# An attention and two-FFN kernel: v transposed by VectorE in blocks of 32, four H banks, FFN2's weights in 16 pieces

## The reference

```python
def reference(q, k, v, tau, moe_w_in, moe_w_out, moe_a, moe_b, moe2_w_in, moe2_w_out):
    # q, k, v: [1, 6016, 256]; w_in: [256, 2048]; w_out: [2048, 256]; all float32
    qn = q / (norm(q, axis=1) + 1e-6); kn = k / (norm(k, axis=1) + 1e-6)
    s = kn.transpose(0, 2, 1) @ qn / tau              # 256 x 256, over the channels
    a = exp(s - s.max(-1)); a /= a.sum(-1) + 1e-9
    x = (v @ a).reshape(6016, 256)
    h = x @ moe_w_in                                  # first FFN (FFN1)
    P = a0 + a1*h + a2*h**2 + a3*h**3
    Q = 1.0 + abs(b0)*abs(h) + abs(b1)*h**2
    x = (P / (Q + 1e-6)) @ moe_w_out
    h = x @ moe2_w_in                                 # second FFN (FFN2)
    return (h * clip(h + 3, 0, 6) / 6) @ moe2_w_out
```

## Time and profile before

| what | value |
|---|---|
| median of three executions | 1181.27 us |
| profiled execution, its time | 1181.6 us |
| its span, first to last instruction | 1179.4 us |
| mean granted TensorE clock | 0.988 of full speed |
| busy share of the span | PE 97%, weight loads 83%, DVE 74%, ACT 75%, POOL 64% |
| chain that ended last | PE 92%, DVE 3%, ACT 2%, POOL 1%, issue 1% |
| start (q, k, softmax, first fold piece) | 0 to 64.9 us |
| step 0 (FFN1 of block 0 alone) | 64.9 to about 134 us |

### The profile page before, as it was taken

How to read it: one execution, slowest core, us unless ns; L and a number is a source line. 1 busy time by engine, 2 the same in 40 slices (tenths; PEclk the granted TensorE clock), 3 DMA queues, 4 the chain that set the end, 5 groups by cost and what they waited for, 6 DMA issues and landing times.

```text
span 1179.4 us, 17866 instructions
## 1 busy us (share of the span) xinstructions
PE 1140.6 (97%) x6058; PEld 975.1 (83%) x6058; DVE 877.7 (74%) x1258; ACT 880.1 (75%) x1463; POOL 749.6 (64%) x596
## 2 busy tenths in 40 slices
PE   7887799999999999999999999999999999999998
PEld 6765688888888888888888888888888888888887
DVE  6768888877877877777777777777787777777721
ACT  6577788877777777777777777777787787787743
POOL 2157567766666666666666666666666666666643
PEclk9889999999999999999999999999999999999999
DMA  9731000000000000000000000000000000000000
GB/s 320 277 123 34 1 1 19 15 1 19 1 19 19 1 19 19 2 19 19 1 18 19 2 19 18 1 18 19 1 19 18 1 19 1 1 19 1 1 18 18
DMA packets 15961, 34.19 MB, mean 29 GB/s; under 512 B 1792, under 2 KB 6144, under 8 KB 15616
## 3 DMA queue, kind: packets, MB, share of 16 engines
q1 hardware_dynamic: 15872, 33.04, 7.8%
HBM read 26.87 MB, written 6.16 MB: 28 GB/s over the span
## 4 chain that ended last, share of the span: by engine, by line
PE 92%; DVE 3%; ACT 2%; POOL 1%; issue 1%; DMA 0%; SPq 0%; POOLq 0%; DVEq 0%; ACTq 0%
PE H L367 15%; PE H L369 14%; PE H L368 14%; PE OP L491 7%; PE OP L493 7%; PE OP L495 7%; PE YP L367 7%; PE YP L368 7%; PE YP L369 7%; PE OP L376 4%; DVE SQ L783 1%; PE H L407 1%; POOL SQ L324 1%; PE OP L430 1%; DVE g_hi L776 1%
## 5 line engine op out<-in xcount | busy, mean ns | idle before, releaser
L324 POOL TENSOR_TENSOR SQ<-SQ,AB 128x512 f32<-128x512 f32 (+1 forms) x192 | 244.5, 1273 | 360.5 <-ACT SQ L586 320.3
L336 POOL TENSOR_TENSOR g_lo<-R,g_hi 128x512 fp32r<-128x512 f32 (+1 forms) x192 | 246.1, 1282 | 28.6 <-ACT g_hi L617 28.6
L584 ACT ACTIVATE AB<-H,absb 128x512 f32<-128x512 f32 (+1 forms) x192 | 130.3, 679 | 158.1 <-PE H L369 156.9
L330 POOL TENSOR_TENSOR g_lo<-SQ,Y 128x512 fp32r<-128x512 f32 (+1 forms) x192 | 245.1, 1277 | 1.7 <-DVE SQ L791 1.7
L491 PE MATMUL OP<-wd_hi,g_hi 128*128 128x256 f32 x752 | 211.9, 282 | 0.6 <-POOL g_lo L336 0.6
L493 PE MATMUL OP<-wd_lo,g_hi 128*128 128x256 f32 x752 | 211.8, 282 | 0.0
L761 DVE TENSOR_TENSOR T<-T,H 128x512 f32<-128x512 f32 (+1 forms) x192 | 129.5, 674 | 108.8 <-ACT T L592 108.8
L495 PE MATMUL OP<-wd_hi,g_lo 128*128 128x256 f32 x752 | 209.6, 279 | 0.0
L776 DVE SCALAR_TENSOR_TENSOR g_hi<-H,coef,Y 128x512 fp32r<-128x512 f32 (+1 forms) x192 | 141.9, 739 | 76.0 <-ACT Y L605 75.7
L367 PE MATMUL YP<-g_hi,wd_hi 128*128 128x512 f32 (+1 forms) x384 | 154.4, 402 | 14.0 <-POOL g_lo L330 12.1
L611 ACT ACTIVATE R<-H 128x512 f32<-128x512 f32 (+1 forms) x192 | 113.6, 591 | 69.8 <-PE H L369 68.6
(11 more groups left out here) (83 smaller groups left out, 2188.7 us busy)
## 6 DMA issues: line engine op xcount, KB each, us to landing
qk<-in_q SPq DMA_DIRECT2D x23, 256.0 KB, 7.1
qk<-in_k SPq DMA_DIRECT2D x23, 256.0 KB, 8.2
v_raw<-in_v SPq DMA_DIRECT2D x11, 512.0 KB, 3.5
out<-o_tok SPq DMA_DIRECT2D x11, 512.0 KB, 2.6
w_raw_b<-in_moe_w_out SPq DMA_DIRECT2D x8, 512.0 KB, 6.1
w_raw_a<-in_moe_w_in SPq DMA_DIRECT2D x1, 2048.0 KB, 13.0
w_raw_b<-in_moe_w_in SPq DMA_DIRECT2D x4, 512.0 KB, 6.9
v_raw<-in_v SPq DMA_DIRECT2D x1, 384.0 KB, 13.5
```

The source lines that it names most:

```text
L324: nc.gpsimd.tensor_tensor(SQ[:, j % 4, 0:w], SQ[:, j % 4, 0:w], AB[:, j % 2, 0:w], ALU.add)\
L330: nc.gpsimd.tensor_tensor(g1_lo[:, j % 4, 0:w], SQ[:, j % 4, 0:w], Y[:, j % 2, 0:w], ALU.mult)\
L336: nc.gpsimd.tensor_tensor(g2_lo[:, j % 4, 0:w], R[:, j % 4, 0:w], g2_hi[:, j % 4, 0:w].bitcast(fp32), ALU.subtract).then_inc(g2_lo_done, 1)
L584: nc.scalar.activation(AB[:, j % 2, 0:w], h, ACT.Abs, scale=absb[:, 0:1])
```

## The change

- **v.** `load_v` brings a block in eight transfers of 32 partitions, in runs of 32 floats (128 bytes), so that each 32x32 square lies where the square of the transposed block belongs. `v_transpose` then transposes inside the squares, one VectorE instruction for 128x512, SBUF to SBUF, in chunks 5 and 8 (`V_AT`). ACT makes `vT_hi`, POOL `vT_lo`. TensorE's `transpose_v`, the two places in the ring and DVE's `vT_split` go. Also for block 0: its transposes now come after the copy of probT on DVE.
- **Banks.** One tile `H` with four banks. FFN1 takes banks 0 and 1, FFN2 banks 2 and 3; in step 0 FFN1 has all four. `up1` of chunk j waits for `rest` of chunk j-2, `up2` for `gate2` of chunk j-2.
- **Lags.** `LAG_DOWN1` is 3 (was 2), so `SHIFT2` is 4 (was 3).
- **Weights.** FFN2's weights have their own buffers and are split in 16 pieces of 128x512, in slots of steps 0 and 1 (slot = 16 t + j). Their loads wait for no split, and stand behind block 1 of v in SP's queue. `PIECES` is eight folds of 256 columns (was 2 of 256 and 3 of 512).
- **GpSimd's order in a chunk.** `q_body(j)`, `g2_split`, `vT_split`, a piece of weights, `quotient_lo(j-1)`. The wait for `product` is gone. `R` has two buffers (was four).
- Tokens of a block are stored in rows of 128 tokens, not four neighbours to a partition.

```diff
-    LAG_DOWN1 = 2
+    LAG_DOWN1 = 3
-    V_BEHIND = 7, 10
-    W_SLOTS = 0, 6
-    RING = 3
+    V_AT = 5, 8
+    WU2_AT = 2, 6, 10, 11, 12, 13, 15, 23
+    WD2_AT = 14, 16, 17, 18, 19, 27, 29, 30
-    PIECES = [2, 2, 4, 4, 4]
+    PIECES = [2] * 8
-        R = sb("R", [P, 4, W], fp32)
+        R = sb("R", [P, 2, W], fp32)
-        H1, H2, YP, OP = ps("H1", RING), ps("H2", 1), ps("YP", 2), ps("OP", 2)
+        H, YP, OP = ps("H", 4), ps("YP", 2), ps("OP", 2)
...
+        def h1(t, j):
+            turn = 4 if isinstance(t, int) and t == 0 else 2
+            return H[:, j % turn, 0:width(t)]
+
+        def wait_h1(engine, t, j):
+            if isinstance(t, int) and t == 0:
+                if j >= 4:
+                    wait_chunk(engine, rest_done, (0, j - 4))
+            elif isinstance(t, int) and t == 1 and j < 2:
+                wait_chunk(engine, rest_done, (0, J - 4 + j))
+            else:
+                wait_chunk(engine, rest_done, back(t, j, 2))
...
             def load_v(blk):
                 m = width(blk) // P
-                sp.wait_ge(vT_psum, CT * blk)
-                sp.dma_start(v_raw[:, 0:m, :], tokens_of(v[0], blk, m)).then_inc(v_in, 16)
+                sp.wait_ge(vT_done, CT * blk)
+                rows = tokens_of(v[0], blk, m).rearrange("(a q) (h b r) -> h b q a r", q=32, h=CT, b=4)
+                to = v_blocks[:, :, 0:m * P].rearrange("p h (a r) -> p h a r", r=32)
+                for c in range(CT):
+                    for b in range(4):
+                        sp.dma_start(to[32 * b:32 * (b + 1), c], rows[c, b]).then_inc(v_in, 16)
...
             sp.dma_start(w_raw_a[:], w_up_h[0]).then_inc(w1_in, 16)
-            sp.dma_start(v_raw[:, 0:tiles_of[0], :], tokens_of(v[0], 0, tiles_of[0])).then_inc(v_in, 16)
+            load_v(0)
             load_v(1)
-            for k in (1, 2):
-                for part in range(4):
-                    load_weight(k, part)
+            for part in range(4):
+                load_wu2(part)
+            for part in range(4):
+                load_wd2(part)
...
+            def vT_split(blk, c, par):
+                w = width(blk)
+                pool.wait_ge(vT_hi_done, CT * blk + c + 1)
+                low_half(vT_lo[par][:, c, 0:w], vT_raw[par][:, c, 0:w], vT_hi[par][:, c, 0:w]).then_inc(vT_lo_done, 1)
...
             def step(t, par):
                 for j in range(J):
-                    y = stage(t, j - LAG_DIVIDE)
                     if exists(t):
-                        if y:
-                            wait_chunk(pool, product_done, y)
                         q_body(t, j)
-                    if y:
-                        quotient_lo(*y)
                     if x := stage(t - 1, j - SHIFT2):
                         g2_split(*x)
-                    if isinstance(t, int) and t == 0:
-                        for k in (1, 2):
-                            if W_SLOTS[k - 1] <= j < W_SLOTS[k - 1] + 4:
-                                weight_lo(k, j - W_SLOTS[k - 1])
+                    if j in V_AT and exists(t) and exists(t + 1):
+                        vT_split(t + 1, V_AT.index(j), 1 - par)
+                    if slot(t, j) in WU2_AT:
+                        wu2_split(WU2_AT.index(slot(t, j)))
+                    if slot(t, j) in WD2_AT:
+                        wd2_split(WD2_AT.index(slot(t, j)))
+                    if y := stage(t, j - LAG_DIVIDE):
+                        quotient_lo(*y)
...
-                for i in range(m):
-                    done = nc.tensor.transpose(H1[:, b, i * P:(i + 1) * P], v_raw[:, i, c * P:(c + 1) * P], ident[:])
-                done.then_inc(vT_psum, 1)
...
+            def v_transpose(blk, c, par):
+                w = width(blk)
+                if c == 0:
+                    dve.wait_ge(v_in, 128 * (blk + 1))
+                    if exists(blk - 2):
+                        wait_chunk(dve, u1_done, (blk - 2, J - 1))
+                nc.vector.transpose(vT_raw[par][:, c, 0:w], v_blocks[:, c, 0:w]).then_inc(vT_done, 1)
 
             dve.wait_ge(probT_psum, 1)
             nc.vector.tensor_copy(probT, YP[:, :, 0:C]).then_inc(probT_ready, 1)
             for c in range(CT):
-                vT_split(0, c, 0)
+                v_transpose(0, c, 0)
...
             def step(t, par):
                 for j in range(J):
+                    if j in V_AT and exists(t) and exists(t + 1):
+                        v_transpose(t + 1, V_AT.index(j), 1 - par)
                     if j == LAG_DOWN1 and exists(t - 1):
                         yT_split(t - 1)
```

More of the change, by code:

```diff
@@ L103, in attention_ffn_ffn @@
         small = sb("small", [P, 48], fp32)
[L104 to L106 removed]
+        v_blocks = sb("v_blocks", [P, CT, W], fp32)
         o_tok = sb("o_tok", [P, BT, C], fp32)
@@ L145, in attention_ffn_ffn @@
         w1_in, v_in = map(sem, ("w1_in", "v_in"))
-        wb_in = [sem(f"wb_in_{i}") for i in range(4)]
+        wd1_in, wu2_in, wd2_in = ([sem(f"{x}_in_{i}") for i in range(4)] for x in ("wd1", "wu2", "wd2"))
         ident_ready, ones_ready, absb_ready = map(sem, ("ident_ready", "ones_ready", "absb_ready"))
@@ L210, in every_step, with wait_h2, wu2_unit, wd2_unit @@
                 body(t, t % 2)
[L213 to L237, removed]
-        def h2(blk, j):
-            last = isinstance(blk, int) and blk == NB - 1
-            return (H1 if last and j % 2 else H2)[:, 0, 0:width(blk)]
+        def h1(t, j):
[9 more added lines that the diff above has]
+                wait_chunk(engine, rest_done, back(t, j, 2))
+        def h2(blk, j):
+            return H[:, 2 + j % 2, 0:width(blk)]
+        def wait_h2(engine, blk, j):
+            if isinstance(blk, int) and blk == 0 and j < 2:
+                wait_chunk(engine, rest_done, (0, J - 2 + j))
+            else:
+                wait_chunk(engine, g2_done, back(blk, j, 2))
+        def wu2_unit(u):
+            at = u // 2 % 2 * F + u // 4 * (F // 2) + u % 2 * UNIT
+            return slice(at, at + UNIT)
+        def wd2_unit(u):
+            return slice(u * UNIT, (u + 1) * UNIT)
+        def slot(t, j):
+            return t * J + j if isinstance(t, int) else None
         def stage(t, at):
@@ L436, in up1 @@
                 w = width(t)
-                wait_bank(pe, t, place(j))
+                wait_h1(pe, t, j)
                 if j == 0:
@@ L463, in up2 @@
                 w = width(blk)
-                if at := back(blk, j, 2 if isinstance(blk, int) and blk == NB - 1 and j else 1):
-                    wait_chunk(pe, g2_done, at)
-                if j == 0 and isinstance(blk, int) and blk == 0:
-                    pe.wait_ge(split_lo, 8)
+                wait_h2(pe, blk, j)
+                if isinstance(blk, int) and blk == 0 and j in (0, J // 2):
+                    pe.wait_ge(wu2_lo_done, 4 if j == 0 else 8)
                 cols = slice(j * P, (j + 1) * P)
@@ L591, in p_start @@
                 wait_chunk(act, t3_done, back(t, j, 2))
-                nc.scalar.activation(T[:, j % 2, 0:w], H1[:, bank(place(j)), 0:w], ACT.Identity, bias=A2, scale=A3)\
+                nc.scalar.activation(T[:, j % 2, 0:w], h1(t, j), ACT.Identity, bias=A2, scale=A3)\
                   .then_inc(t_done, 1)
@@ L818, in step @@
                         rest(*x)
-                    if j in V_BEHIND and exists(t) and exists(t + 1):
-                        vT_split(t + 1, V_BEHIND.index(j), 1 - par)
                     if exists(t):
```

166 lines of the change are left out of this document (81 added, 85 removed).

## The result

The changed kernel takes 1162.1 us (median of 4 runs, 1161.0 to 1164.5) against 1181.4 (1180.1 to 1181.5). The ratio is 0.984, 95% interval [0.9825, 0.9859]. The sign was right, the size was not.

What follows compares the result with a forecast made beforehand. PE was taken to bound seven eighths of the profile, step 0's latency chain an eighth. -8.6 - 0.6 - 3.2 + 2.6 = -9.8 took 1181.6 to 1171.8 us; forecast 1166 to 1177 (0.60), range 1163 to 1180.

Steps and rivals of the forecast that it cites:

- the sum for step 0: Step 0: 16 x 3.45 plus 0.8, pieces 8 x 0.45, folds 0.5 x 6, v 1.65; 64.4 us, 3.2 gained.
- The rival that I gave 0.13: Step 0's chain gets shorter if `product` and `q_body` don't exclude each other: step 60 us, time 1163 to 1167; chance 0.13.
- Transposes off PE: Steps 1 to 10: 20 groups of four transposes leave PE, 0.43 us each, 8.6 us gained.
- FFN2's bank: FFN2's two banks: `up2` no longer waits for the `gate2` right before; half of PE's 1.25 us wait, 0.6 us gained.
- Two banks cost nothing in the loop: FFN1 on two banks in the loop: 2.75 us of slack before `up1` takes up the delays of `rest`; cost 0.
- The lags: One more chunk passes before PE is full: cost 2.6 us, bounds 0 and 5.
- The start: Before the first `up1`: v's new path is done by 63 us and hidden by 1.9 us; no cost.
- The small packets: v's loads in packets of 128 bytes: 6 to 50 ns each, 25 taken, nothing lost.
- the rival of the late v: v's packets over 50 ns lengthen ACT's wait in chunk 2; from 93 ns on the kernel is slower; chance 0.05.
- `q_body` first makes it slower: Step 0 and ramp: a late DVE finds `q_body` running and loses 1.0 us, 4.0 a chunk; 1185.5 us; chance 0.10.
- The start didn't eat the gain: Rival: ACT's stall, the dear ramp and late v eat the gain; 1176 to 1180 us; chance 0.10.
- the mean clock: Rival: PE at its lower clock in step 0, or two banks binding in the loop; each up to 10 us; chance 0.02.

Runs made afterwards that it cites:

- e1: The changed kernel with GpSimd's wait for `product` before `q_body` put back in all steps; 1162.75 us, ratio 0.9850 to the kernel before.
- e2: The kernel before without GpSimd's wait for `product`, nothing else changed; 1177.67 us, ratio 0.9973.
- e5: The kernel before with v alone changed: square blocks, VectorE's transpose, `vT_lo` on POOL, no v transposes on TensorE; 1175.02 us, ratio 0.9945.
- e6: The kernel before with `LAG_DOWN1` 3 in place of 2 (so `SHIFT2` 4); 1181.97 us, ratio 1.0012.
- e7: The changed kernel with FFN1 on four H banks also in the first four chunks of step 1; 1163.30 us, ratio 0.9855 to the kernel before.
- e10: The changed kernel with the wait for `product` put back from step 1 on, not in step 0; 1161.21 us, ratio 0.9834 to the kernel before.
- e11: The changed kernel with `LAG_DOWN1` 2 in place of 3 (`SHIFT2` 3); 1198.76 us, ratio 1.0156 to the kernel before.
- e9: The kernel before with v by VectorE, 16 half pieces of weights in slots 2 to 17, and no wait for `product`; 1165.92 us, ratio 0.9876.
- e4: The kernel before with FFN2's weights in 16 half pieces, one in each chunk of step 0; 1174.32 us, ratio 0.9951.

## Why the prediction was right in sign and too small

The sum was made against the profiled execution, and so is this. Forecast -9.8, measured -20.0 in time and -19.8 in span. Of the 10 us that were missing, 7.15 are in step 0, 1.4 in the start, and 1.4 in all that follows step 0.

**The step that failed is the sum for step 0** ("8 x 0.45", "0.5 x 6", "1.65" on a base of "16 x 3.45"): 64.4 us forecast, 57.25 measured. Two parts, told apart by e1:

- *The extras don't add.* I priced a piece on POOL, a fold on DVE and v on both as if each came alone, and added the prices: 9.2 us over 55.2. In e1, with the chunk of 3.45 that I assumed, they came to 58.45 - 55.2 = 3.25. That is 5.95 us. A chunk with a fold and a piece is 3.72. That `product` asks 0.4 us before POOL is done was a right reading, but it loses only 0.27 by it, and the fold's 0.4 us on DVE falls into the same time: in a chunk that has both it is spent once.
- *The plain chunk is 3.2, not 3.45.* I argued that `product` asks before `q_body` anyhow, so that dropping the wait changes nothing. e2 (3.2 in plain chunks of the old kernel) and e1 against after (1.2 us of step 0) show that it does. The order was right, the conclusion was not: I took the exclusion of the two for as long as the wait. `q_body` in second place lost 0.08 us to the exclusion where the wait had put it off by 0.3, and the chunk shrank to the loop of ACT and POOL. Behind folds and v, DVE is late, `q_body` comes first, and from about 80 us on DVE sets the pace (38.4 of 40 us busy from 80 to 120, against 36.6 in e1, and over 60% of the chain that ended last is DVE's from 66 to 130; by the lengths of `product` about 3.0 and 0.9 of these are its waiting for POOL).

The rival that I gave 0.13 comes nearest: it had ACT and POOL setting the pace, then DVE, at 3.0 to 3.1 us a chunk. But I hung it on a condition that is false, that the two don't exclude each other: one `product` of 1.65 us and one of 1.41 are in the trace. They exclude each other, and it costs only their overlap, a mean of 0.26 over 16 (0.819 us against 0.56). Its 60 us for the step was still too long, since it too added up the extras.

**Transposes off PE: -8.6.** The mechanism is right, the size a bit too large: e5 gives 0.375 for a group, 7.5 for the 20. I had read a difference of 0.43 between two stretches of a single chunk; the length of a whole step, which e5 shows, holds two groups and everything around them, and is the better measure. Steps 2 to 11 became 11.5 us shorter: 7.0 as in e5, 2.6 as in e6, and about 2 that no run explains. The changed kernel's steps 8 to 10 take 89.49 us each, 0.3 less than e5's 89.81, while e7 and e10, with nearly its code, have 89.70. The four executions of the changed kernel are 3.6 us apart, so part of the 2 us may be only that.

**FFN2's bank: -0.6.** PE's wait of 1.25 us is gone entirely, so it was under-sized by 0.65. e6, without the banks, still has 1.2 us of it.

**Two banks cost nothing in the loop.** Right: PE waits for none there. One wait of 5.1 us in the ramp is theirs, and e7 shows that it covers another of nearly the same length.

**The lags: +2.6.** Measured alone +1.4 by the runs, +0.4 by the span (e6), inside my bounds of 0 and 5. Without the 1.9 us of idle PE that the lag removed there, it would be 2.3 by the span, near the forecast: that the forecast came out too dear is owed to a gain that I didn't know of. In the changed kernel step 1 is 0.3 longer and the tail 3.2, with part of the loop's 11.5 as its counterpart. What I did not weigh is that the lag is needed: e11 puts its absence at 37 us.

**The start: 0.** v's path was hidden, as forecast: the first `up1` waits for a fold, as in the earlier trace rows. The 1.4 us by which it is earlier lie within what the start varies by. These are the changed kernel's DVE, POOL and PE in the start:

```profile
58.41 1.02 DVE L748 STREAM_TRANSPOSE vT_raw<-v_blocks 128x384 f32<-128x384 f32 x2
```

```profile
59.62 1.96 POOL L331 TENSOR_TENSOR vT_lo<-vT_raw,vT_hi 128x384 fp32r<-128x384 f32 x2 [15.03 <-ACT vT_hi L563]
```

```profile
63.51 0.66 PE L398 MATMUL H<-vT_hi,wf_hi 128*128 128x384 f32 x1 [1.18 <-DVE wf_lo L758]
```

POOL is ready at 61.6, 1.9 us before `up1`, exactly the slack forecast.

**The small packets.** A block of 4096 packets took at most (0.48 + 0.19) x 16 x 5 = 53.6 us of DMA engine time in the two windows above, 13 ns a packet; my bounds were 6 and 50, my value 25. So the rival of the late v (0.05, from 93 ns) had no ground. The page "DMA: Bandwidth & Descriptors" of the Trainium skill, section "Specifications", wants 512 bytes for line rate, and the trace agrees: 1 KB took 50 ns, an eighth of that is 6, and a packet took 13. The factor is 2, and it is hidden.

**`q_body` first makes it slower (0.10).** In step 0 `q_body` does come first where DVE is late, and costs `product` 0.4 to 0.85 us in five of 16 chunks (in a sixth the piece behind it costs 1.1), but at most 0.1 in the others. DVE did stay late, as this rival said, but at 57.25 / 16 = 3.6 us a chunk, folds and all, not 4.0.

**The other rivals.** The start didn't eat the gain, ACT waits for none of FFN2's weights in the changed kernel, and the mean clock was 0.990 against 0.988.

Not separated: what banks, lags, folds, POOL's order and slots do to each other. e9 leaves 3.8 us for them together.

## What to carry to other kernels

When a chunk gets several extra pieces of work, list them by engine and take the longest engine's or chain's new length, not the sum of their prices; check a sum of that sort by one chunk of the old trace that already has two of them. Before pricing a removed wait at nothing because the two instructions exclude each other anyhow, ask how much of the wait the exclusion really replaces: here 0.08 us of 0.3. Splitting work on a side engine in halves can pay without moving any of it away (16 halves in the same step, 5.9 us), and a longer lag that costs 1 us alone can be what the rest of a change stands on.

## What the runs showed of the hardware that was not expected

- `product` on VectorE and an instruction of GpSimd that exclude each other lose their overlap less about 0.15 us, whichever comes second. `product` lost 0.09 for 0.23 of overlap (103.27), 0.26 for 0.41 (e4), 0.85 for 1.00 (84.98), 1.09 for 1.23 (114.23) and 1.36 for 1.51; on GpSimd, `q_body` lost 0.08 for 0.23 (e2), and a half piece behind `product` 0.23 for 0.36 (1.52 us instead of 1.29, at 103.56).
- VectorE's transpose of 128x512 fp32 in squares of 32 takes 0.706 us, the same as a `tensor_tensor` of that size (0.69), and 128x384 takes 0.55.
- 128-byte packets took at most 13 ns of DMA engine time each, twice what bytes alone say.
- An idle time of PE with no visible cause (0.8 and 1.1 us in two steps of the loop of the kernel before) is there in every kernel with `LAG_DOWN1` 2 and gone or at most 0.5 us in every one with 3.
- `product` at 128x512 has a mean of 0.69 us in the kernel before and 0.785 in e5, which changes only v and keeps the wait; e1 has 0.80 and the changed kernel 0.81. The wait doesn't protect it from what else POOL does.
